# Fewer operations in the centroid chain, head 0's loads on other queues, and the first softmax inverse on VectorE alone

## What is computed

```python
q_n = q / (np.linalg.norm(q, axis=-1, keepdims=True) + 1e-06)
k_n = k / (np.linalg.norm(k, axis=-1, keepdims=True) + 1e-06)
c_n = centroids / (np.linalg.norm(centroids, axis=-1, keepdims=True) + 1e-06)
q_assign = np.argmax(np.einsum('bhsd,hcd->bhsc', q_n, c_n), axis=-1)
k_assign = np.argmax(np.einsum('bhsd,hcd->bhsc', k_n, c_n), axis=-1)
mask = q_assign[:, :, :, None] == k_assign[:, :, None, :]
scores = np.where(mask, scale * np.matmul(q, k.transpose(0, 1, 3, 2)), -1000000000.0)
attn = np.exp(scores - np.max(scores, axis=-1, keepdims=True))
attn = attn / (np.sum(attn, axis=-1, keepdims=True) + 1e-09)
x = matmul(attn, v), heads joined to 512 columns, 1536 tokens
h = x @ w_in;  P = a0 + a1 h + a2 h^2 + a3 h^3;  Q = 1 + |b0||h| + |b1| h^2
x = (P / (Q + 1e-06)) @ w_out
out = (silu(x @ w_gate) * (x @ w_val)) @ w_out2
```

## Time and profile before

| | us |
|---|---|
| median of 3 runs | 779.73 |
| lowest, highest | 779.42, 779.96 |
| the profiled execution, its own time | 780.16 |
| its span | 778.3 |
| TensorE busy in the span | 772.1 (99%) |
| VectorE, ScalarE, GpSimd busy | 565.0, 522.0, 522.8 |

### The profile page before, as it was taken

How to read it: one execution, slowest core, us unless ns; L and a number is a source line. 1 busy time by engine, 2 the same in 40 slices (tenths; PEclk the granted TensorE clock), 3 DMA queues, 4 the chain that set the end, 5 groups by cost and what they waited for, 6 DMA issues and landing times.

```text
span 778.3 us, 12686 instructions
## 1 busy us (share of the span) xinstructions
PE 772.1 (99%) x4219; PEld 699.2 (90%) x4219; DVE 565.0 (73%) x1010; ACT 522.0 (67%) x996; POOL 522.8 (67%) x457
## 2 busy tenths in 40 slices
PE   8999999999999999999999999999999999999998
PEld 8899999999998888888888888899999999999997
DVE  6999999999998787777777777644544555554554
ACT  6889888988888787686767789553554444333322
POOL 5679999997575997222222488879888975665610
PEclk9999999999999999999999999999999999999999
DMA  8757665463402600000000111342212204111002
GB/s 187 189 147 182 165 176 139 118 163 91 120 14 82 189 1 1 1 0 1 1 0 1 28 44 39 95 122 55 55 28 55 55 29 135 55 41 42 27 1 82
DMA packets 57521, 57.53 MB, mean 74 GB/s; under 512 B 6576, under 2 KB 44272, under 8 KB 57456
## 3 DMA queue, kind: packets, MB, share of 16 engines
q1 hardware_dynamic: 57296, 56.32, 27.0%
q10 hardware_dynamic: 160, 0.39, 0.2%
HBM read 33.59 MB, written 3.15 MB: 47 GB/s over the span
## 4 chain that ended last, share of the span: by engine, by line
PE 97%; ACT 1%; DVE 1%; DMA 0%; issue 0%; ACTq 0%
PE ps L1344 19%; PE ps L1346 19%; PE ps L1345 19%; PE ps L1499 8%; PE ps L1518 4%; PE ps L1520 4%; PE ps L1442 4%; PE ps L1443 4%; PE ps L1441 4%; PE ps L1487 4%; PE ps L1473 4%; PE ps L1552 2%; ACT prob L917 1%; PE ps L1451 0%; DMA cen<-in_centroids 0%
## 5 line engine op out<-in xcount | busy, mean ns | idle before, releaser
L609 POOL TENSOR_TENSOR den<-den,mag 128x512 f32<-128x512 f32 x48 | 62.3, 1298 | 118.5 <-ACT den L790 118.3
L668 POOL TENSOR_TENSOR w_lo<-w_raw,w_hi 128x768 fp32r<-128x768 f32 (+1 forms) x48 | 101.7, 2127 | 56.4 <-ACT w_hi L849 56.4
L1346 PE MATMUL ps<-x_hi,w_lo 128*128 128x512 f32 (+1 forms) x384 | 139.4, 363 | 0.0
L1344 PE MATMUL ps<-x_hi,w_hi 128*128 128x512 f32 (+1 forms) x384 | 139.1, 362 | 0.0
L1345 PE MATMUL ps<-x_lo,w_hi 128*128 128x512 f32 (+1 forms) x384 | 139.1, 362 | 0.0
L1251 DVE TENSOR_TENSOR probT_lo<-ps,probT_hi 128x384 fp32r<-128x384 f32 x192 | 97.8, 551 | 9.4 <-ACT probT_hi L937 8.2
L690 POOL TENSOR_SCALAR prob<-prob,row_inv 128x768 f32<-128x768 f32 x96 | 85.7, 907 | 27.7 <-DVE row_inv L1241 26.7
L937 ACT ACTIVATE probT_hi<-ps 128x384 fp32r<-128x384 f32 x192 | 83.5, 487 | 17.9 <-PE ps L1499 15.1
L1230 DVE TENSOR_REDUCE neg_max<-ps 128x1 f32<-128x768 f32 x96 | 90.7, 946 | 2.0 <-PE ps L1487 1.5
L917 ACT ACTIVATE prob<-ps,neg_max 128x768 f32<-128x768 f32 x96 | 86.6, 902 | 2.1 <-DVE neg_max L1230 2.0
L1499 PE MATMUL ps<-ident,prob 128*128 128x128 f32 x576 | 79.8, 274 | 0.3 <-DVE probT_lo L1251 0.3
(11 more groups left out here) (150 smaller groups left out, 1990.6 us busy)
## 6 DMA issues: line engine op xcount, KB each, us to landing
w_raw<-in_moe_w_gate SPq DMA_DIRECT2D x48, 128.0 KB, 2.3
w_raw<-in_moe_w_val SPq DMA_DIRECT2D x48, 128.0 KB, 2.6
k_hihi<-qk_hi SPq DMA_DIRECT2D x31, 192.0 KB, 3.3
w_raw<-in_moe_w_in SPq DMA_DIRECT2D x16, 256.0 KB, 3.7
w_raw<-in_moe_w_out SPq DMA_DIRECT2D x16, 256.0 KB, 4.5
qk_raw<-in_q SPq DMA_DIRECT2D x16, 192.0 KB, 4.0
qk_low<-qk_hi SPq DMA_DIRECT2D x16, 192.0 KB, 3.7
qk_low<-qk_lo SPq DMA_DIRECT2D x16, 192.0 KB, 4.1
```

The lines of the kernel that those rows point to most:

```text
L668: did(g.tensor_tensor(lo[:, wave, :], raw[:, wave, :], hi[:, wave, :].bitcast(F32), ALU.subtract), s_w2lo)
L1344: mm(dst, hi, m_hi, start=start, stop=False)
L1346: return mm(dst, lo, m_hi, start=False, stop=stop)
```

## The change

Four edits, all in the first 20 us or so of the program, and one constant:

1. The centroids go out on ScalarE's DMA queue, ahead of k of head 0; SyncE's queue begins with q of head 0.
2. The centroid chain: the square root takes a small constant (1e-36, a new memset on VectorE, semaphore `s_guard`) as its bias, so the guard operation goes. Multiply and add become one operation. Four operations on a column are left of six, and `cen_hh` is written by VectorE where ScalarE did it.
3. The first denominator (one column) is no longer made by ScalarE: VectorE reduces the two values of `row_sum` (the sum, and the epsilon beside it) itself, under a semaphore of its own, `s_den_0`.
4. At step 3 the inverse of columns 1 and 2 stands behind `sum_logit` of head 2 instead of ahead of it.
5. `WARM_CEN` is 14 instead of 19.

```diff
-    WARM_CEN, WARM_CENT, WARM_LOGIT, WARM_TOP = 19, 6, 4, 5
+    WARM_CEN, WARM_CENT, WARM_LOGIT, WARM_TOP = 14, 6, 4, 5
@@ SyncE
-            sp.dma_start(cen[:, :], centroids.rearrange("h c d -> (h c) d")).then_inc(s_cen_in, 16)
             sp.dma_start(*load_sides(0)[0]).then_inc(s_qk_in[0], 16)
@@ ScalarE
+            sc.dma_start(cen[:, :], centroids.rearrange("h c d -> (h c) d")).then_inc(s_cen_in, 16)
             sc.dma_start(*load_sides(0)[1]).then_inc(s_qk_in[0], 16)
             sc.wait_ge(s_cen_v, 2)
-            s.activation(cs[:, 1:2], cs[:, 0:1], ACT.Sqrt).then_inc(s_cen_a, 1)
+            sc.wait_ge(s_guard, 1)
+            s.activation(cs[:, 1:2], cs[:, 0:1], ACT.Sqrt, bias=cs[:, 6:7]).then_inc(s_cen_a, 1)
             s.preload_act_table_set("natural_log_exp_and_others")
-            sc.wait_ge(s_cen_v, 8)
-            s.activation(cen_hh[:, 0:3:2, :].bitcast(F32R), cen[:, :].unsqueeze(1).to_broadcast([P, 2, D]),
-                         ACT.Identity, scale=cs[:, 7:8]).then_inc(s_cen_hh, 1)
@@ ScalarE, denominators
-                if half is not None:
+                if half is not None and cols.stop > 1:
                     sc.wait_ge(s_eps, 1)
-                    sc.wait_ge(s_exp, HALF * (half + 1) if half else cols.stop)
+                    sc.wait_ge(s_exp, HALF * (half + 1))
@@ VectorE
+            v_.memset(cs[:, 6:7], SQUARE_MIN).then_inc(s_guard, 1)
             ve.wait_ge(s_cen_a, 1)
-            then(v_.tensor_scalar(cs[:, 2:3], cs[:, 1:2], 1e-30, None, ALU.max))
-            then(v_.reciprocal(cs[:, 3:4], cs[:, 2:3]))
-            then(v_.tensor_tensor(cs[:, 4:5], cs[:, 0:1], cs[:, 3:4], ALU.mult))
-            then(v_.tensor_tensor(cs[:, 5:6], cs[:, 4:5], cs[:, 1:2], ALU.add))
-            then(v_.tensor_scalar(cs[:, 6:7], cs[:, 5:6], 0.5, EPS_NORM, ALU.mult, ALU.add))
-            then(v_.reciprocal(cs[:, 7:8], cs[:, 6:7]))
+            then(v_.reciprocal(cs[:, 2:3], cs[:, 1:2]))
+            then(v_.scalar_tensor_tensor(out=cs[:, 3:4], in0=cs[:, 2:3], scalar=cs[:, 0:1], in1=cs[:, 1:2],
+                                         op0=ALU.mult, op1=ALU.add))
+            then(v_.tensor_scalar(cs[:, 4:5], cs[:, 3:4], 0.5, EPS_NORM, ALU.mult, ALU.add))
+            then(v_.reciprocal(cs[:, 5:6], cs[:, 4:5]))
+            v_.tensor_scalar(cen_hh[:, 0:3:2, :].bitcast(F32R), cen[:, :].unsqueeze(1).to_broadcast([P, 2, D]),
+                             cs[:, 5:6], None, ALU.mult).then_inc(s_cen_hh, 1)
@@ VectorE, inverses
-                    ve.wait_ge(s_den, n)
+                    if cols.stop == 1:
+                        ve.wait_ge(s_eps, 1)
+                        ve.wait_ge(s_exp, 1)
+                        v_.tensor_reduce(row_den[:, cols], row_sum[:, cols, :], AX.X, ALU.add).then_inc(s_den_0, 1)
+                        ve.wait_ge(s_den_0, 1)
+                    else:
+                        ve.wait_ge(s_den, half + 1)
                     v_.reciprocal(row_inv[:, cols], row_den[:, cols]).then_inc(s_inv, 1)
@@ VectorE, the step loop
-                late = step > T
+                late = step > T or step == FIRST_DEN + 1
...
                     sum_logit(h)
+                    if step == FIRST_DEN + 1:
+                        inverses(step)
                     top_logit(h)
```

More of the change, by code:

```diff
@@ L51, in build_program @@
     BIG = 2.0 ** 96
-    EPS_NORM, EPS_SUM = 1e-6, 1e-9
+    EPS_NORM, EPS_SUM, SQUARE_MIN = 1e-6, 1e-9, 1e-36
     DEN0 = 1.0 + 1e-6
@@ L238, in build_program @@
         "s_zeros", "s_gap", "s_topz", "s_scale", "s_const", "s_row0", "s_par", "s_bneg", "s_eps", "s_early"))
+    s_guard = sem("s_guard")
     s_cen_a, s_cen_v, s_cen_hh, s_cen_ll, s_cen_t, s_cen = (sem(x) for x in (
@@ L244, in build_program @@
         "s_logit", "s_top", "s_istop", "s_topT", "s_topT_in", "s_rank", "s_cluster"))
-    s_score, s_max, s_exp, s_den, s_inv, s_norm = (sem(x) for x in (
-        "s_score", "s_max", "s_exp", "s_den", "s_inv", "s_norm"))
+    s_score, s_max, s_exp, s_den, s_den_0, s_inv, s_norm = (sem(x) for x in (
+        "s_score", "s_max", "s_exp", "s_den", "s_den_0", "s_inv", "s_norm"))
     s_pT, s_pT_hi, s_pT_lo, s_pv, s_xhi, s_xlo = (sem(x) for x in (
@@ L1080, in _ @@
                                     in0=cen[:, :].unsqueeze(1).to_broadcast([P, 2, D]),
-                                    scalar=cs[:, 7:8], in1=cen_hh[:, 0:3:2, :],
+                                    scalar=cs[:, 5:6], in1=cen_hh[:, 0:3:2, :],
                                     op0=ALU.mult, op1=ALU.subtract).then_inc(s_cen_ll, 1)
@@ L1235, in inverses @@
                 if half is not None:
-                    n = inverse_count(half, cols)
                     if half >= 2:
                         ve.wait_ge(s_norm, HALF * (half - 1))
-                    ve.wait_ge(s_den, n)
+                    if cols.stop == 1:
[5 more added lines that the diff above has]
+                        ve.wait_ge(s_den, half + 1)
                     v_.reciprocal(row_inv[:, cols], row_den[:, cols]).then_inc(s_inv, 1)
@@ L1290, in _ @@
                     top_logit(h)
-                if late:
+                if late and step > T:
                     inverses(step)
```

## The result

The changed kernel is slower, by little: median 780.13 us of 22 runs (779.70 to 785.40) against 779.67 of 22 of the kernel before (779.31 to 780.20), ratio 1.0018 with a 95% interval of 1.0009 to 1.0026. I had forecast 779.06. The times have two parts. Seventeen of the 22 lie between 779.70 and 780.27 (0.46 above before by the medians), one at 781.16 (mean granted clock 0.998; before has such runs too, up to 781.00 in the later rounds), and four between 784.95 and 785.40; no run of before came near those. The ratio counts the four, so it is above the 1.0006 of the medians. The profiled execution took 779.86 with a span of 778.1, before 780.16 with 778.3.

A forecast was written before the change was run, and what follows sets the result against it. TensorE bounds the kernel (97% of the chain), so only its start-up waits in the first 27 us could yield; 0.55 from the centroid chain plus 0.12 from the inverses, 0.67 off the 779.73 median, gave 779.06 us, range 778.3 to 780.4.

The forecast's parts named there:

- the clock: Start-up: TensorE's faster level was expected at much the same time despite 0.9 us idle; a later rise was a rival, 0.10.
- The gain forecast for the start: First 27 us: 0.55 us from the centroid chain and 0.12 from the inverses, 0.67 in all.
- The centroid chain: Start-up: VectorE writes `cen_hh`, ScalarE's table load sets the limit, `cenT` comes at 6.46 instead of 7.01: 0.55 us.
- The queue edit: First loads: costed at nothing, no gain in the centroids' landing at 3.41; plus or minus 0.3 us possible.
- They are on nobody's path, so nothing is won or lost by their time: Warm-ups before the transposes: removing five only leaves TensorE idle from about 4.5 to 5.4, at no gain or loss.
- I expect it to come at much the same time: TensorE's rise to the faster level, there by 6.7 us before: not delayed by 0.9 us of idle time.
- the rival: Clock rises later, logits and warm-ups run slower: 781.7 to 782.4, or 780.1 to 780.4 if only head 0's; chance 0.10.
- A later difference that changes after 27 us, where I expect none: Sign of being wrong: every later row should be earlier by the same 0.67 us, to the end.
- The inverses: First and second inverse, early steps: a gain of 0.12 us, both ends -0.01 and 0.18.
- The last copy of head 0: SyncE's copy before the first score: 0.26 us of cover left; if later, up to 0.24 us of the gain lost.
- The loads: q and k of head 0 on swapped queues: k lands at 4.55 to 5.45, in time for ScalarE's 5.46, barely.
- the third rival: Loads or last copy of head 0 come late and eat 0.2 to 0.7 us: 779.3 to 779.8; chance 0.18.

The follow-up runs named there:

- E10: E7 with the first loads queued as in the kernel before: 779.64 us, ratio 1.0003, two of 11 late.
- E2: The kernel before with 14 warm-ups instead of 19: ratio 1.0030; five runs at 779.32 to 779.75, seven at 783.79 to 784.94.
- E4: The kernel before with the centroid chain edits alone: 779.60 us, ratio 1.0000.
- E6: The kernel before with one memset more on VectorE, in its idle time at about 1.5 us: 780.73 us, ratio 1.0015.
- E11: The changed kernel with 32 added instructions on VectorE, long-met waits at about 541 us: 780.06 us, ratio 1.0011, two of 12 late.
- E5: The changed kernel with the guard's memset on GpSimd instead of VectorE: 779.10 us, ratio 0.9995.
- E3: The kernel before with the new order of loads alone: 779.47 us, ratio 0.9996.
- E7: E5 with 16 warm-ups before the transposes instead of 14 and 7 after them instead of 6: 779.04 us, ratio 0.9994.
- E1: The changed kernel with 19 warm-ups instead of 14: 780.33 us, ratio 1.0008, none of 11 late.
- E9: E7 with 10 warm-ups ahead of the transposes instead of 16: 783.28 us, ratio 1.0044, all five late.
- E12: E8 with the added VectorE memset of E6: 779.21 us, ratio 1.0012, four of 12 late.
- E8: The changed kernel without its edits of the first two inverses: 779.41 us, ratio 1.0013, three of 12 late.

## Why the prediction was wrong

Two terms were put at nothing and were not: the place of later instructions in VectorE's longer program (1.2 us by the profiles) and the clock (5 us in 4 of 22 runs). The gain forecast for the start was sound as far as the runs tell.

**The centroid chain** was right in its mechanism. The four column operations, `cen_hh` at 0.28, ScalarE as the new limit behind its table load: all are in the profile. Its size was read from one execution, though. The 3.41 of the centroids' landing is one of two values: with the old order of loads the profiles have `cen_sq` at 3.43 twice (before, E10) and at 2.49 to 2.71 three times (E2, E4, E6); with the new order it is at 2.48 to 2.83 in all nine. Most of the 1.21, and of the 1.42 at 27 us, is the luck of these two profiles. E6 has before's chain and 19 warm-ups with an early landing, and starts at 19.45; the changed kernel, E11 and E5 start at 18.92, 19.25 and 19.39. The moment of the clock's rise is a second draw: 5.2 us in the changed kernel's profile, the earliest of all, 5.6 in E6 and 7.4 in E4, which starts at 19.98 although its transposes start at 5.38 as in E6. The queue edit, which I costed at nothing, may make the landing steadier, but two of five against none of nine does not show it; what that is worth by itself was not resolved (E3: 0.9996, with 1.0 inside; E10 is 0.04 under its before and E7, with the new queue, 0.41 under its own).

**"They are on nobody's path, so nothing is won or lost by their time"**, of the warm-ups, failed. It held only for the late landing. When the centroids land at 2.5, 19 warm-ups hold TensorE until 5.58 and the shorter chain waits for it: E1's start is 0.71 later than the changed kernel's, of which 0.57 is there at the transposes (5.39 against 4.82). Part of the chain's gain comes through all the same (E4, about 0.3), so the fewer warm-ups let more of it through, and are worth something, by the five runs of E2 that are not late 0.32.

**"I expect it to come at much the same time"**, of the clock's rise, failed as well, and so did the form of the rival. I gave it 0.10 and priced it as a case in which every run is late by 2 to 3 us. It is a mixture: 4 of 22 runs, each 5 us late, since the level stayed low not until the ranks at 8 to 12 us but, in the late profiles, to 15.6 to 17.0, and everything before that is stretched. In the mean this is 4/22 x 5.1 = 0.9 us, more than my whole gain. It was luck that it was not worse: I had forecast 0.9 us of idle time before the transposes, and the early landing left 0.30. With 0.77 (E2) seven of 12 were late, with 1.21 (E9) all five. E9 and E1 bracket it: ten warm-ups, all late; 19, none. The Trainium skill ("TensorE: Matmul & The Clock Gate", Part 1, "The HAM clock gate") says that the moment of the rise varies from run to run; the runs agree, and I should have made the rival a share of the runs and not a yes or no.

**"A later difference that changes after 27 us, where I expect none"**: this is the step that turned the sign of the median. I counted what each added instruction costs where it stands, and the guard's memset stands in idle time, so it was free. What I did not count is that it makes VectorE's program one instruction longer. Every later instruction then lies at another place of the 8 KB pieces in which the program is fetched. E5 and E6 show by one memset each, in both directions, what this costs here: 0.3 us in the middle and 0.91 in the tail, 1.2 together. All runs move: E6 lies at 780.32 to 781.27 and before, beside it, at 778.86 to 780.50, the medians 1.28 apart. The changed kernel is 1.03 above E5, or 0.81 when each is taken against before in its own rounds. The 0.91 is tied to the fetch itself: moved to 756 in E11, it leaves the tail at 3.23. For the steps at 555 and 29 us the table and E12 show that they go with the program's length; that a crossing from one piece to the next costs 0.2 to 0.35 us where VectorE has no slack is my reading, and it fits that the fetch starts in the records 0.66 to 0.74 us behind the delayed instruction in all five profiles that have such a step (after, E1, E4, E6, E8). Why 8 KB in the stores' way cost 0.9 us is open.

**The inverses**: 0.18 against my 0.12, the upper end. **The last copy of head 0** cost nothing in the changed kernel's profile: its first score, at 11.62, follows the transpose before it by 0.18 us, as it does in before (12.68 to 12.86). **The loads**: q or k of head 0 did hold ScalarE's first half in some profiles, by 0.26 in E1 and E4, 0.20 in E8, 0.18 in E9 and 0.30 in E11, part of the third rival.

**The sum as it was.** Median: +1.2 from the program's length, and so about -0.75 from the start, against my 0.67; together +0.46. Taken from E5 and E7, which lack the 1.2, the start is worth 0.35 to 0.41 of the medians. The same sum for E8, E11 and E12 (before's median in their rounds, less the median of their runs that are not late, plus what their middle and tail have over 754.75 and 3.23, plus 0.18 where the inverses' edits are missing) gives 0.57, 0.78 and 0.88. These are estimates. Before's level moved by 0.3 between sets of runs, so they are not in conflict; the five with 14 warm-ups and the short chain (after, E5, E8, E11, E12) have a mean of 0.67, which is what I had forecast for the start. The late runs come on top.

## What to carry to other kernels

An instruction added in idle time is not free by that alone: it shifts all that follows it in the engine's program against the fetches, so look for an instruction fetch inside the last stores, and try the instruction on another engine before judging the edit. Warm-up matmuls have two prices, the time in which they hold up the first real work and the share of executions in which the faster level comes late; size them so that TensorE doesn't idle at the typical landing of the first load, and count late runs among twenty or more: E5 showed none in 11, with the changed kernel's warm-ups. One profile gives one draw of a DMA's landing; where a term hangs on it, carry both values. The moment of the clock's rise is such a draw as well.

## What of the hardware was unexpected

- An 8 KB instruction fetch that falls into the final stores made the end 0.91 us later (tail 4.14 against 3.23; E5, E6, E11), and steps of 0.2 to 0.35 us in mid-kernel come and go with one instruction. The Trainium skill ("Runtime: NRT & Kernel Launch", "Instruction fetch mechanics") has such fetches in 16 KB blocks and their cost mostly hidden; here those of one queue (q14) are 8 KB each and those of another (q8) 16 KB, and one of 8 KB was not hidden where it fell into the stores.
- A late execution holds TensorE at the lower level until 15.6 to 17.0 us, 128x64 matmuls 0.21 apart instead of 0.11, and costs 4.2 to 5.1 us by the medians of each kernel's late and other runs. With 14 warm-ups and, by the profiles, 0.3 to 0.5 us of idle time ahead of the transposes it came in 13 of 69 runs; before, with 19 warm-ups and 0.42 us in its profile, had none in 132. In the executions that are not late the rise still came anywhere from 5.2 to 7.4 us.
- The same 32 KB load landed at 2.5 to 2.8 or at 3.4 us, depending on the execution.
- Waits that are long met are not free: 32 of them took VectorE at most the 3.0 us up to 543.91 in E11, so up to 0.09 each.
